# Attention with a fused MLP and expert stage on one core: from the seventh head pair on, the three engines take two attention steps at a time and the MLP groups go whole

## What is computed

```python
# q, k, v: (4, 8, 576, 64); blocks of 64
scores = scale * np.matmul(q, k.transpose(0, 1, 3, 2))
scores = np.where(block_i >= block_j, scores, -1000000000.0)
attn = np.exp(scores - max); attn = attn / (sum + 1e-09)
x = (attn @ v), heads side by side        # (2304, 512)
h = x @ w_in                              # (512, 2048)
x = np.maximum(0.01 * h, h) @ w_out       # (2048, 512)
# then: skip score, gate over 8 experts, top 1, y = gate * relu(x @ w1[e]) @ w2[e], out = x + y
```

## Time and profile before

| | |
|---|---|
| time, median of 3 runs (lowest, highest) | 786.27 us (786.05, 786.92) |
| the profiled execution: its time, its span | 787.97 us, 786.2 us |
| mean granted TensorE clock | 0.998 |
| busy: PE, DVE, ACT, POOL | 761.7, 368.5, 301.4, 148.8 us |
| PE's share of the chain that ended last | 91% |
| copies of MLP groups on ACT (L977) | x96, 491 ns each |

### The profile page before, as it was taken

The page is one execution under the profiler, slowest core; times in us unless marked ns, Lnnn a source line. Parts: engine busy times, 40 slices in busy tenths (PEclk is TensorE's granted clock), DMA queues, the critical chain, the costliest instruction groups (busy, mean ns, idle before and its releaser), DMA issues.

```text
span 786.2 us, 13538 instructions
## 1 busy us (share of the span) xinstructions
PE 761.7 (97%) x4738; PEld 643.4 (82%) x4738; DVE 368.5 (47%) x771; ACT 301.4 (38%) x711; POOL 148.8 (19%) x193
## 2 busy tenths in 40 slices
PE   7999989999999998999999999999999999999997
PEld 3555878888888887999987877878778879999996
DVE  5667455543343554013355554555554342444644
ACT  4566655544444554234432222222221131333533
POOL 3226564221121231100020000000000031222222
PEclk9999999999999999999999999999999999999999
DMA  4344767554444541365665656556462038777750
GB/s 125 96 126 142 211 197 201 160 143 130 118 137 128 147 116 57 93 214 162 191 174 177 196 150 190 144 178 189 142 192 68 28 114 246 234 226 236 235 172 4
DMA packets 97671, 121.68 MB, mean 155 GB/s; under 512 B 14226, under 2 KB 60578, under 8 KB 97608
## 3 DMA queue, kind: packets, MB, share of 16 engines
q1 hardware_dynamic: 94776, 116.50, 50.4%
q0 software_dynamic: 2080, 3.77, 1.5%
q10 hardware_dynamic: 752, 0.59, 0.2%
HBM read 89.35 MB, written 31.57 MB: 154 GB/s over the span
## 4 chain that ended last, share of the span: by engine, by line
PE 91%; ACT 2%; issue 2%; SPq 1%; DVE 1%; DMA 1%; POOL 1%; DVEq 0%; POOLq 0%; ACTq 0%
PE ps_hid L1731 10%; PE ps_h L1520 9%; PE ps_x L1573 9%; PE ps_x L1575 8%; PE ps_x L1574 8%; PE ps_h L1522 8%; PE ps_h L1521 8%; PE ps_o L1502 5%; PE ps_t L1476 4%; PE ps_y L1743 3%; PE ps_y L1744 3%; PE ps_y L1742 3%; PE ps_s L1427 2%; PE ps_s L1463 2%; PE ps_s L1464 1%
## 5 line engine op out<-in xcount | busy, mean ns | idle before, releaser
L1520 PE MATMUL ps_h<-xh,win_h 128*128 128x384 f32 x384 | 136.5, 355 | 3.1 <-ACT act L977 2.4
L1522 PE MATMUL ps_h<-xh,win_l 128*128 128x384 f32 x384 | 128.9, 336 | 0.0
L1521 PE MATMUL ps_h<-xl,win_h 128*128 128x384 f32 x384 | 128.8, 335 | 0.0
L1573 PE MATMUL ps_x<-wout_h,g_hi 128*128 128x512 f32 x288 | 117.0, 406 | 0.0
L1575 PE MATMUL ps_x<-wout_h,g_lo 128*128 128x512 f32 x288 | 112.5, 391 | 0.0
L1574 PE MATMUL ps_x<-wout_l,g_hi 128*128 128x512 f32 x288 | 112.2, 390 | 0.0
L977 ACT ACTIVATE act<-ps_h 128x384 f32<-128x384 f32 x96 | 47.1, 491 | 154.9 <-PE ps_h L1522 154.9
L965 ACT ACTIVATE prob<-ps_s,neg_max 128x128 f32<-128x128 f32 (+3 forms) x144 | 78.6, 549 | 28.2 <-DVE neg_max L1126 27.6
L1132 DVE COPY pt<-ps_t 128x384 f32<-128x384 f32 (+4 forms) x113 | 48.4, 436 | 82.4 <-PE ps_t L1476 82.1
L1166 DVE TENSOR_TENSOR g_lo<-g_raw,g_hi 128x512 fp32r<-128x512 f32 x72 | 49.5, 688 | 78.0 <-ACT g_hi L987 77.9
L1126 DVE TENSOR_REDUCE neg_max<-ps_s 128x1 f32<-128x128 f32 (+3 forms) x144 | 71.8, 504 | 30.4 <-PE ps_s L1430 15.3
(11 more groups left out here) (185 smaller groups left out, 1053.0 us busy)
## 6 DMA issues: line engine op xcount, KB each, us to landing
w_sb<-in_w SPq DMA_DIRECT2D x64, 512.0 KB, 5.4
hidden<-act SPq DMA_DIRECT2D x96, 192.0 KB, 2.3
g_raw<-hidden SPq DMA_DIRECT2D x72, 256.0 KB, 4.1
k_raw<-in_k_t SPq DMA_DIRECT2D x40, 144.0 KB, 3.1
x2rows<-x SPq DMA_DIRECT2D x18, 256.0 KB, 2.3
out<-x SPq DMA_DIRECT2D x18, 256.0 KB, 2.6
w_stage<-in_w_in SPq DMA_DIRECT2D x16, 256.0 KB, 3.4
w_stage<-in_w_out SPq DMA_DIRECT2D x16, 256.0 KB, 2.8
```

Source lines behind the costliest of these rows:

```text
L1520: e.matmul(dst, win_h[:, f, kc, :], xh[slot][:, kc, :], start=kc == 0, stop=False)
L1521: e.matmul(dst, win_h[:, f, kc, :], xl[slot][:, kc, :], start=False, stop=False)
L1522: last = e.matmul(dst, win_l[:, f, kc, :], xh[slot][:, kc, :], start=False, stop=kc == KC - 1)
L1573: e.matmul(dst, hi, wout_h[:, f, :], start=f == 0, stop=False)
```

## The change

The loops of PE, ACT and DVE are split at step 54 (`ROW_UNITS`, the seventh pair). Up to there they are as before, but a group of the MLP is no longer cut in two. From there they go by s, s + 1. `groups_at` takes the groups of both steps and deals them out in front of and behind the transposes (a single one goes behind). `turn_inverse` moves behind the second lot and now always waits for the first half of the output to be copied.

ACT and DVE run ahead by two steps in this order: ACT copies the groups in front, does the exponentials of s + 2 and s + 3 (a unit with i = 8 that stands at s + 3 is put off to the next round), turns copies, then `between(s + 2)` and `between(s + 3)` with `high_q`, `high_x` and `high_w_in`, and last copies the groups behind. SP and POOL keep their loops; `fill_steps` gives SP slightly other steps for storing groups.

```diff
     at = {s: [] for s in range(STEPS)}
     for g in range(N_ATT_HID):
-        for part in range(2):
-            n = 2 * g + part
-            if g < FC:
-                s = 50 + 34 * n // (2 * FC)
-            elif g < 3 * FC:
-                s = 86 + 34 * (g - FC) // (2 * FC)
-            elif g < TWO_BANKS:
-                s = 122 + 22 * (n - 6 * FC) // (2 * (TWO_BANKS - 3 * FC))
-            else:
-                s = N_UNITS + 5 + g - TWO_BANKS
-            at[s].append((g, part))
+        if g < FC:
+            s = 50 + 34 * g // FC
+        elif g < 3 * FC:
+            s = 86 + 34 * (g - FC) // (2 * FC)
+        elif g < TWO_BANKS:
+            s = 122 + 22 * (g - 3 * FC) // (TWO_BANKS - 3 * FC)
+        else:
+            s = N_UNITS + 5 + g - TWO_BANKS
+        at[s].append(g)
     return at
...
-    return [g for g, part in FILL.get(s, ()) if part]
+    return FILL.get(s, ())
+
+
+def groups_at(s):
+
+    groups = FILL[s] + FILL[s + 1]
+    return groups[:len(groups) // 2], groups[len(groups) // 2:]
...
+                if i == UNITS - 1:
+                    add_epsilon(p)
...
-            for s in range(STEPS):
+            def between(s):
                 p, i = divmod(s, UNITS)
-                if 3 <= s < N_UNITS + 3 and (s - 3) % UNITS in by_act((s - 3) // UNITS):
-                    copy_turned(s - 3)
-                for g in filled_at(s - 1):
-                    copy_hidden(g)
-                if s < N_UNITS:
-                    exponential(s)
...
-                if i == 8 and p < N_PAIRS:
-                    add_epsilon(p)
-            for g in filled_at(STEPS - 1):
-                copy_hidden(g)
...
+            for s in range(ROW_UNITS, STEPS, 2):
+                before, behind = groups_at(s)
+                for g in before:
+                    copy_hidden(g)
+                if s + 1 < N_UNITS and behind_tail(s + 1):
+                    exponential(s + 1)
+                if s + 2 < N_UNITS:
+                    exponential(s + 2)
+                for u in (s - 2, s - 1):
+                    if u < N_UNITS and u % UNITS in by_act(u // UNITS):
+                        copy_turned(u)
+                if s + 3 < N_UNITS and not behind_tail(s + 3):
+                    exponential(s + 3)
+                between(s + 2)
+                between(s + 3)
+                for g in behind:
+                    copy_hidden(g)
...
-                if i == 0 and 1 <= p <= N_PAIRS:
+                if i == (0 if p < ROW_PAIRS else 1) and 1 <= p <= N_PAIRS:
                     invert(p - 1)
-                if i == 2 and 1 <= p <= N_PAIRS:
+
...
+            for s in range(ROW_UNITS, STEPS, 2):
+                for u in (s + 2, s + 3):
+                    if u < N_UNITS:
+                        maximum(u)
+                for u in (s - 2, s - 1):
+                    if u < N_UNITS and u % UNITS not in by_act(u // UNITS):
+                        copy_turned(u)
+                for u in (s, s + 1):
+                    p, i = divmod(u, UNITS)
+                    part = p_v_at(u)
+                    if part and part[3] == (QT if part[1] else 2):
+                        copy_o(part[0], part[1])
+                    if i == 1 and 1 <= p <= N_PAIRS:
+                        copy_inverse(p - 1)
+                between(s + 2)
+                between(s + 3)
...
-                if p < ROW_PAIRS:
-                    e.wait_ge(s_of, 2 * p + 1)
+                e.wait_ge(s_of, 2 * p + 1)
...
-                if part == 0:
-                    hidden_waits(g)
-                for kc in range(KC // 2 * part, KC // 2 * (part + 1)):
+                hidden_waits(g)
+                for kc in range(KC):
                     e.matmul(dst, win_h[:, f, kc, :], xh[slot][:, kc, :], start=kc == 0, stop=False)
                     e.matmul(dst, win_h[:, f, kc, :], xl[slot][:, kc, :], start=False, stop=False)
                     last = e.matmul(dst, win_l[:, f, kc, :], xh[slot][:, kc, :], start=False, stop=kc == KC - 1)
-                if part:
-                    last.then_inc(s_h, 1)
+                last.then_inc(s_h, 1)
...
+            for s in range(ROW_UNITS, STEPS, 2):
+                for u in (s + 2, s + 3):
+                    if u < N_UNITS:
+                        scores(u)
+                before, behind = groups_at(s)
+                for g in before:
+                    hidden(g)
+                for u in (s - 2, s - 1):
+                    if u < N_UNITS:
+                        transposes(u)
+                products_with_v(s)
+                products_with_v(s + 1)
+                for g in behind:
+                    hidden(g)
+                for u in (s, s + 1):
+                    p, i = divmod(u, UNITS)
+                    if i == 1 and ROW_PAIRS <= p <= N_PAIRS:
+                        turn_inverse(p - 1)
```

More of the change, by code:

```diff
@@ L1029, in _, with behind_tail @@
                     high_w_in(f)
-                if i == 8 and p < N_PAIRS:
-                    add_epsilon(p)
-            for g in filled_at(STEPS - 1):
-                copy_hidden(g)
+            for s in range(ROW_UNITS + 2):
+                if s >= 3 and s - 3 < ROW_UNITS - 2 and (s - 3) % UNITS in by_act((s - 3) // UNITS):
+                    copy_turned(s - 3)
+                if s <= ROW_UNITS:
+                    for g in filled_at(s - 1):
+                        copy_hidden(g)
+                exponential(s)
+                between(s)
+            def behind_tail(u):
+                return (u - P_RING) % UNITS == TAIL
+            for s in range(ROW_UNITS, STEPS, 2):
[14 more added lines that the diff above has]
+                for g in behind:
+                    copy_hidden(g)
             e.wait_ge(s_h, N_ATT_HID)
@@ L1167, in low_g, with between @@
                                 g_hi[j % G_RING][:, :, :].bitcast(F32), ALU.subtract).then_inc(s_glo, 1)
-            scale_q(0)
-            for s in range(STEPS):
+            def between(s):
                 p, i = divmod(s, UNITS)
[L1172 to L1175, removed]
                 if i == 4 and p + 1 < ROW_PAIRS:
@@ L1186, in _ @@
                     low_q(2 * p + 1)
-                if i == 0 and 1 <= p <= N_PAIRS:
+                if i == (0 if p < ROW_PAIRS else 1) and 1 <= p <= N_PAIRS:
                     invert(p - 1)
-                if i == 2 and 1 <= p <= N_PAIRS:
+            scale_q(0)
+            for s in range(ROW_UNITS + 2):
+                maximum(s)
+                if s >= 3 and s - 3 < ROW_UNITS - 2 and (s - 3) % UNITS not in by_act((s - 3) // UNITS):
+                    copy_turned(s - 3)
+                between(s)
+                p, i = divmod(s, UNITS)
+                if i == 2 and p >= 1:
                     copy_inverse(p - 1)
@@ L1508, in turn_inverse, with hidden @@
                 e.wait_ge(s_inv, p + 1)
-                if p < ROW_PAIRS:
-                    e.wait_ge(s_of, 2 * p + 1)
+                e.wait_ge(s_of, 2 * p + 1)
                 e.transpose(ps_o[0:UNITS, B_COLS:B_COLS + P], inv[:, :], ident[:, :]).then_inc(s_invp, 1)
-            def hidden(g, part):
+            def hidden(g):
                 m, f = divmod(g, FC)
@@ L1539, in hidden_waits, with products_with_v @@
                     e.wait_ge(s_act, g)
[L1541 to L1546, removed]
+            def products_with_v(s):
                 p, i = divmod(s, UNITS)
@@ L1549, in _ @@
                     p_v(*p_v_at(s))
-                if i == 1 and 1 <= p <= N_PAIRS:
+                if i == 1 and 1 <= p <= ROW_PAIRS - 1:
                     turn_inverse(p - 1)
+            scores_of_both(0)
+            for s in range(ROW_UNITS):
+                if ROW_UNITS <= s + 2:
+                    scores(s + 2)
+                if s >= 2:
+                    transposes(s - 2)
+                products_with_v(s)
+                p, i = divmod(s, UNITS)
                 if i in GROUP_AT:
@@ L1555, in _ @@
                         scores_of_both(n)
-                for g, part in FILL[s]:
-                    hidden(g, part)
+                for g in FILL[s]:
+                    hidden(g)
[9 more added lines that the diff above has]
+                        transposes(u)
+                products_with_v(s)
+                products_with_v(s + 1)
+                for g in behind:
+                    hidden(g)
+                for u in (s, s + 1):
+                    p, i = divmod(u, UNITS)
+                    if i == 1 and ROW_PAIRS <= p <= N_PAIRS:
+                        turn_inverse(p - 1)
             for g in range(N_ATT_HID, N_HID):
-                for part in range(2):
-                    hidden(g, part)
+                hidden(g)
             def project(k):
```

## The result

The changed kernel takes 795.41 us (median of 4 runs, 794.83 to 796.07), the kernel before 786.42 (786.05 to 786.92) on the same chip: a ratio of **1.0114**, 95% interval 1.0097 to 1.0132. It is slower by 9.0 us; forecast were 5.0 more, with 783.5 to 799 as range. The 6.9 us between the spans are what a trace can place.

A forecast was written before the change was run, and what follows sets the result against it. TensorE was taken as the bound, only its waits counting. Part 1 -1.5, dense stretch +5.4, early +1.6 and late -0.5 sum to +5.0: median 786.27 to 791.3 us, own range 788 to 796, wider range 783.5 to 799.

The forecast's parts named there:

- ACT held by `high_q`, dense: Groups 16 to 47, pairs 10 and 12: `high_q` awaiting next-round scores holds the group's copy, four times 1.3, 5.3 us.
- Rival 1: ACT is not held: each hold by `high_q` and `high_x` costs little; sum -4.6, 781.7 us; chance 0.14.
- ACT late through `high_x`, dense: Groups 16 to 47: `high_x` and exponentials in front of the copy, 0.65 in even and 0.39 in odd pairs, 2.0 us.
- The short waits: Groups 16 to 47: waits between groups with only transposes (2.6 us) or only scores, ACT free (1.0 us), between them.
- Part 1, fewer changes: Fewer changes from transposes to MLP matmuls, roughly 92 such places halved: -1.5 us, ends 0 and -2.3.
- the priced 0.11: Behind transposes a group's second matmul starts 0.28 us after its first instead of 0.17, 0.11 more there.
- Part 3, early: Groups 2 to 15, one a round: waits of 8.6 us against 7.0 in the kernel before, +1.6; ends -3 and +8.
- rival 2: Early steps take more: `high_w_in`, also in front of the copy, and late keys give +8 instead of +1.6; 797.7; chance 0.15.
- The holds by `high_q`, priced at 4.0: Early steps, pairs 6 and 8: `high_q` in front of the copy, about 1.15 (tail) and 0.85, 4.0 us.
- The 2.6 for the keys: Early steps: pair 7's tail, already waiting 1.47 for keys, asked for a step (2.4 us) earlier; 2.6 us of waiting.
- Part 4, late: Late steps: one held copy (1.15, pair 14) and about 1.0 in rounds without a group, against 2.7: -0.5 us.
- halves become whole groups and add nothing: Halved MLP groups become whole ones at the same places, with no gain or loss of their own: 0.

The follow-up runs named there:

- e1: Changed kernel with ACT's copy of the groups behind moved in front of the second step's `between`, still behind the first's; 789.12 us, ratio 1.0034.
- e2: Changed kernel with ACT's copy of the groups behind moved in front of both steps' `between`; 787.20 us, ratio 1.0000.
- e4: Kernel before, one step at a time, with only the filling changed to whole MLP groups; 785.15 us, ratio 0.9982.
- e11: Changed kernel with the odd head's keys copied earlier on SP's queue, for steps under 86 only; 795.73 us, ratio 1.0108.
- e5: e2 with the odd head's keys copied ahead of the loads of V and the next head on SP's queue; 784.02 us, ratio 0.9976.
- e3: Changed kernel with rounds of two steps begun only at step 86 on all three engines; 790.99 us, ratio 1.0064.
- e3b: e3 with e2's order on ACT, copies in front of both steps' extra work; 782.47 us, ratio 0.9956.
- e7: e4 with the odd head's keys copied ahead of the loads of V and the next head on SP's queue; 785.20 us, ratio 0.9988.
- e10: e4 with the odd head's keys copied earlier on SP's queue, for steps under 86 only; 782.37 us, ratio 0.9932.
- e8: e2 with the odd head's keys copied earlier on SP's queue, for steps under 86 only; 782.15 us, ratio 0.9937.
- e9: e3b with the odd head's keys copied earlier on SP's queue, for steps under 86 only; 782.12 us, ratio 0.9935.

## Why the prediction was right, and where it was not

The direction, the mechanism and the range held; the size was short by 4 us by medians, and by 1.9 us by the profiled executions on which the sum was made.

- **ACT held by `high_q`, dense** (5.3 for four): right in place, number and size. Four waits of 1.23 us in pairs 10 and 12, each with a q rounding in front; removing them gave 4.9. Rival 1 is out.
- **ACT late through `high_x`, dense** (2.0): wrong, it is near 0: e1, with every second `high_x` still in front of the copy, and e2, with none, have the same 108.3, and what after has over e1 is the four holds.
- **The short waits** (2.6 and 1.0): 3.6 forecast, while e2's dense stretch, with no holds, still has 5.1 + 0.7 = 5.8 us of them. The two errors cancel: 10.9 forecast for the stretch, 10.0 + 0.7 measured against the earlier trace rows.
- **Part 1, fewer changes** (-1.5): right in sign. The recorded first products of groups are 359 ns long on average against 368, and with all holds gone the dense stretch takes 108.1 to 108.4 in rounds, 108.8 to 109.0 in single steps: some 0.7 us there, with about equal waits of PEld (6.9 to 7.0 in rounds, 6.8 to 7.1 in single steps). That the priced 0.11 is what was saved is not shown: behind scores, the second matmul of a group is still 0.28 us behind the first at ten of the 15 recorded places of after, and 0.18 to 0.20 at five. The dense stretch as a whole came out at +4.1, with 5.4 less its share of 1.5 forecast.
- **Part 3, early** (+1.6): the step that was undersized, +3.4 measured, or waits of 10.6 us where 8.6 were forecast. `high_w_in` and `high_x`, which stand in front of the copy too, had no price in it. ACT waits 6.8 us for `w_in`, which is rival 2's mechanism at part of its price; and a group is held by 2.4 at 105.7, where `high_x` waits for POOL's normalisation, which no rival named. The holds by `high_q`, priced at 4.0, are two, in pair 8, of 1.04 and 0.72 us (133.91 and 143.91): that error goes the other way. In pair 6 the q rounding's turn comes behind a `w_in` rounding that waits longer. The 2.6 for the keys doesn't follow from the 1.47 and the step of 2.4 beside it (they give 3.9). The wait for pair 7's keys was forecast at 2.6 and is 1.26: TensorE was already late by that hold when it came to the tail.
- **Part 4, late** (-0.5): -0.3, close by luck, since other work makes it up. e4 shows that whole groups gain 1.5 there, which "halves become whole groups and add nothing" had at 0, and the hold in pair 14 (1.0) with the rest takes it back.
- **The range**: its lower end, 783.5, is said to take in most of rival 1, but that rival's own figure, 781.7, lies outside it.

Two rules had been weighed. ScalarE does not pass a waiting instruction: the Trainium skill ("TensorE: Matmul & The Clock Gate", "Architectural detail: the array is 16× 32×32, not 1× 128×128") says it is strictly first in, first out, and e1 agrees, where moving one copy in ACT's order takes away waits of 1.2 us and nothing else. And for part 1 the row gave the right sign, where that page's rule on pulled-ahead loads (part 2, step 1), taken for every matmul, would have made this part 0.

## What to carry to other kernels

When steps are merged into rounds, go through each in-order queue and ask of every instruction that waits what stands behind it: work whose input comes from the next round belongs behind the copy that frees a buffer of this one. Price it for every such instruction, not only the one that was noticed. Where two late things meet in one place, removing one of them can show little (early, 1.2 us in e11 of the 7.1 of both); a single-cause experiment that finds nothing does not clear its cause, and moving a transfer forward only helps as long as its input is there (e5).

## What the runs showed of the hardware

A wait of TensorE can cost more than its length. In e2 the wait for the first keys of a tail ends at 88.8 (1.8 us), that of pair 7 at 109.85 (2.7). Windows around the second (the third number from the end is the granted clock):

```profile
108.00:110.00 2.00, 0.12 (x1) 0.15 (x2) 0.35 (x1) 1.30 (x4) 1.62 (x3) 1.00 0.87 276
110.00:112.00 2.00, 2.00 (x13) 1.86 (x13) 0.76 (x1) 0.00 (x0) 1.11 (x1) 0.75 0.38 114
112.00:114.00 2.00, 2.00 (x11) 1.10 (x10) 0.50 (x2) 1.85 (x5) 0.00 (x0) 0.50 0.69 181
114.00:116.00 2.00, 2.00 (x11) 2.00 (x11) 0.21 (x1) 0.13 (x2) 0.00 (x0) 0.89 0.61 172
```

PE is all but idle up to 110 and busy throughout from there, and yet the clock is at 0.50 of full, its lower level of 1.2 GHz, for a while: 0.50 + 1.00 + 0.22 = 1.7 us are lost. All eight such falls in the profiled executions from 60 to 340 us, in seven kernels, cost 1.7 us each by the same sum. Shortly ahead of each TensorE had waited 1.8 us or more (1.8 and 2.7 in e2, 2.1 in e3, 2.4 in e4, 2.5 in e3b, e7 and e11, 4.4 in e1). After's wait of 2.4, e5's of 2.0 and 1.8 and e10's of 1.8 were followed by none, so a long wait does not always bring one.

The executions without a profile have falls too, as the mean granted clock of each shows, in which 1.7 us are 0.002. (Up to 0.002 more stand for one further fall behind the last matmul, which every trace has and which costs nothing.) Three of e2's 11 have 0.999 or 1.000 and took 784.2 to 785.5 us; the other eight have 0.994 to 0.997 and took 786.9 to 789.9. The two groups are some 3 us apart, which is more than one fall; whether the waits in front were longer too is not shown. After's profiled execution has 0.999, its other three 0.997 and 0.2 to 1.2 us more time, which would fit a fall in each. So part of what e2 lacks against e8 (787.2 to 782.2) is clock, and what moving copies and keys brought by medians is not all waiting time saved. All executions of e8, e9 and e10 have 0.998 or more.
